# Moving the large on-chip buffers of a three-stage kernel to 128-byte boundaries

## What is computed

```python
# attention: a = softmax(q k^T / 8 + bias) over global and local keys; x = a v
# experts (xc: the tokens whose skip score is positive)
logits = xc @ w_gate; e_idx = argmax(logits); gate_w = softmax(logits)[e_idx]
h = np.maximum(xc[mask] @ w1[e], 0.0)            # 512 -> 1024
y[mask] = gate_w[mask, None] * (h @ w2[e])       # 1024 -> 512
out[do_compute] = xc + y
# gated layer
gate = 1.0 / (1.0 + np.exp(-(x @ w_gate)))       # 512 -> 1536
val = x @ w_val
return (gate * val @ w_out).astype(np.float32)   # 1536 -> 512
```

## The kernel before

| buffers | byte of the line before | after |
|---|---|---|
| `w1h`, `w1l`, `w2h`, `w2l`, all of `gat`, `wraw`, `xq` | 32 | 0 |
| `sTh`, `sTl`, `hTh`, `hTl` | 96 | 0 |
| `srow`, `rrow` (start) | 32, 64 | 0, 32 |
| `at_spot`, `lasth` | 32 | 0 |
| `lastl`, `heads_x`, `bias_win`, `bias_0` | 0 | 96 |
| `raw`, `vs`, `score0` to `score2`, `prob0`, `prob1`, `probT0`, `probT1` | 64 | 32 |
| `score3`, `prob2`, `prob3`, `turner` (start) | 32 | 0 |
| `ident`, `before`, `ones` | 0 | 0 |

## Time and profile before

### The profile page before, as it was taken

The page is one execution under the profiler, slowest core; times in us unless marked ns, Lnnn a source line. Parts: engine busy times, 40 slices in busy tenths (PEclk is TensorE's granted clock), DMA queues, the critical chain, the costliest instruction groups (busy, mean ns, idle before and its releaser), DMA issues.

```text
span 954.6 us, 16759 instructions
## 1 busy us (share of the span) xinstructions
PE 942.3 (99%) x5615; PEld 799.3 (84%) x5616; DVE 648.4 (68%) x1497; ACT 510.8 (54%) x1084; POOL 209.8 (22%) x247
## 2 busy tenths in 40 slices
PE   8999999999999999999999999999999999999998
PEld 6888888989999999788888888888888888888887
DVE  7877787755764465686768774777776846766653
ACT  6988898344443243464545564545454634444442
POOL 2415426422111112113232000222210013232100
PEclk9999999999999999999999999999999999999999
DMA  7787875797876274532121343421213431110342
GB/s 260 263 300 270 326 247 187 274 345 278 282 248 230 94 250 164 177 111 66 47 65 47 91 132 127 157 67 45 67 56 93 133 126 58 53 58 12 88 141 91
DMA packets 59660, 146.14 MB, mean 153 GB/s; under 512 B 6336, under 2 KB 12480, under 8 KB 59584
## 3 DMA queue, kind: packets, MB, share of 16 engines
q1 hardware_dynamic: 52624, 120.92, 37.9%
q0 software_dynamic: 6960, 24.27, 7.4%
HBM read 116.77 MB, written 28.40 MB: 152 GB/s over the span
## 4 chain that ended last, share of the span: by engine, by line
PE 91%; DMA 4%; DVE 2%; issue 1%; ACT 1%; SPq 0%; DVEq 0%; POOLq 0%; ACTq 0%
PE bank L2137 35%; PE bank L1866 14%; PE bank L1868 14%; PE bank L1867 13%; PE bank L1882 4%; PE bank L1909 4%; PE bank L1892 3%; PE bank L1925 2%; DMA vs<-in_own_prev_dram 1%; DMA row_table<-pad 1%; PE bank L2065 1%; PE bank L2127 1%; DMA srow<-row_table 1%; ACT prob L1594 1%; DVE score L940 1%
## 5 line engine op out<-in xcount | busy, mean ns | idle before, releaser
L2137 PE MATMUL bank<-xh,ws_h 128*128 128x512 f32 x490 | 190.6, 389 | 0.0
L2137 PE MATMUL bank<-xl,ws_h 128*128 128x512 f32 x490 | 190.6, 389 | 0.0
L2137 PE MATMUL bank<-xh,ws_l 128*128 128x512 f32 x490 | 190.6, 389 | 0.0
L874 POOL TENSOR_TENSOR p<-p,p 128x512 f32<-128x512 f32 x35 | 46.3, 1323 | 388.3 <-DVE p L1495 388.3
L1866 PE MATMUL bank<-woh,hh 128*128 128x512 f32 x288 | 112.9, 392 | 0.0
L1868 PE MATMUL bank<-woh,hl 128*128 128x512 f32 x288 | 112.1, 389 | 0.0
L1867 PE MATMUL bank<-wol,hh 128*128 128x512 f32 x288 | 112.1, 389 | 0.0
L2137 PEld LDWEIGHTS bank<-xh,ws_l 128*128 128x128 f32 x490 | 92.0, 188 | 19.3
L2137 PEld LDWEIGHTS bank<-xl,ws_h 128*128 128x128 f32 x490 | 92.0, 188 | 19.1
L2137 PEld LDWEIGHTS bank<-xh,ws_h 128*128 128x128 f32 x490 | 92.0, 188 | 18.9
L1594 ACT ACTIVATE prob<-score,lowest 128x256 f32<-128x256 f32 (+1 forms) x192 | 91.2, 481 | 6.1 <-DVE lowest L940 6.1
(11 more groups left out here) (272 smaller groups left out, 2018.4 us busy)
## 6 DMA issues: line engine op xcount, KB each, us to landing
wraw<-in_w_dram SPq DMA_DIRECT2D x64, 512.0 KB, 5.5
graw<-in_w_gated_dram SPq DMA_DIRECT2D x36, 512.0 KB, 3.6
woraw<-in_w_out_dram SPq DMA_DIRECT2D x72, 256.0 KB, 2.6
raw<-in_qk_dram SPq DMA_DIRECT2D x48, 336.0 KB, 6.4
vs<-in_own_prev_dram SPq DMA_DIRECT2D x16, 768.0 KB, 5.3
mixed<-xs SPq DMA_DIRECT2D x12, 512.0 KB, 3.2
xq<-mixed SPq DMA_DIRECT2D x12, 512.0 KB, 6.4
out_dram<-ostage SPq DMA_DIRECT2D x22, 256.0 KB, 2.0
```

Source lines behind the costliest of these rows:

```text
L874: pool.tensor_tensor(p7[:], p7[:], p1[:], ALU.add).then_inc(u3_done, 1)
L2137: ins = pe.matmul(bank, w[:, a + k], x[:, q, k], start=(first and k == 0 and i == 0), stop=(k == 1 and i == 2), skip_group_check=not first)
```

## The change

The change moves buffers and nothing else. `SMALL` goes from 7968 to 7936, which is 62 times 128, and so everything that begins at or after it moves 32 bytes down. To make room, `lexp` (216 bytes) leaves the small buffers and gets a place among the attention's; the small buffers behind it move 224 bytes down. The sum of `srow` and `rrow` is rounded up to a multiple of 128 before `sTh`, which puts `sTh`, `sTl`, `hTh` and `hTl` 32 bytes higher than before.

```diff
         UNIT = 8 * KC * FF
-        SMALL = 7968
+        LINE = 128
+        SMALL = 7936
+        assert (BASE + SMALL) % LINE == 0
         SHARED = SMALL + 4 * UNIT
...
         ldiff = small("ldiff", [P, NQ, NE], f32)
-        lexp = small("lexp", [P, NQ, NE + 1], f32)
         lsum = small("lsum", [P, NQ], f32)
...
         place_l = att2("place_l", [P, NQ, 2 * NE + 1], f32)
+        lexp = att2("lexp", [P, NQ, NE + 1], f32)
         so_far = att2("so_far", [P, NQ, NE], f32r)
...
         rrow = moe("rrow", [P, 2, ROW], f32)
+        moe = place(SHARED + 4 * 4 * FF + (4 * 4 * ROW + LINE - 1) // LINE * LINE)
         sTh = moe("sTh", [P, KC, SLOT], f32r)
```

## The result

The changed kernel has a median of 958.1 us (955.9 to 960.3, 20 executions) against 956.6 us (955.3 to 958.1, 20 executions) of the kernel before, measured beside it: ratio 1.0015, 95% interval 1.0008 to 1.0021. It is slightly slower, not faster. The two profiled executions have the same span, 954.6 us, so this difference of 0.15% can't be read from their ends. What the profiles do show is a change in the stretch of the expert phase.

A forecast was written before the change was run, and what follows sets the result against it. From 181 us the matmul engine was taken as the bound: number of matmuls times pitch. Only the second product's -2.56 us counted, all other terms nothing, giving 953.2 us from the median of 955.76 us; range 943 to 958.

The forecast's parts named there:

- the second product's: Experts' 512-column matmuls on `w2h`: pitch to fall 6.67 ns to 226.67 ns, on 384 matmuls 2.56 us saved.
- the first product: Experts' 864 matmuls of 256 columns: relation goes from 64 bytes apart to 0, taken as no change in time.
- the stated end of +2.6 us: First product's slow end: 3 ns more per matmul, if one case of line 2050 carried all its surplus.
- the weight load stands in the way: First product: why 5.8 us less was doubted; a 128-column weight load needs about as long as 256 moving columns.
- The gated layer: Line 2137 and `unit`, 2382 matmuls: both operands move from byte 32 to 0, relation stays, no change; 1 ns is 2.4 us.
- Attention: Its buffers change places in the line; taken as no change, with 1.4 us as the end to either side.
- Nothing changes: Rival: the second product's extra 6.67 ns comes from something other than place in the line; 955.8 us, chance 0.20.
- The start in the line counts by itself: Rival: byte 0 speeds up gated layer and second product by 11.7 us to 944.1 us, far end 916 us; chance 0.20.
- byte 0 is the worse place: Rival: gated layer's weight loads up to 5 ns longer, its pitch 6.67 ns longer, 15.9 us, 971.6 us; chance 0.15.

The follow-up runs named there:

- m1_places: Separate kernel on zeros, not the reference: blocks of 45 matmuls, both operands at byte 0, 32, 64 or 96; same place 226.67 ns at 512 columns, 120.0 ns at 256.
- e3_plus128: Changed kernel with `sTh`, `sTl`, `hTh`, `hTl` 128 bytes higher, distance 0 modulo 256 in both products; ratio 0.9995 to the kernel before.
- experiment 1: The same run as m1_places; its diagonal is the four pairs with both operands at the same place, 226.67 ns at 512 columns.
- Experiment 5: Kernel of m1_places with one stationary operand and the moving one 0 to 1024 bytes further; 226.7 to 234.3 ns at 512 columns, 113.3 to 120.0 ns at 256.

## Why the prediction was wrong

**The step that failed** is the second product's: "After the change `hTh` and `w2h` both stand at byte 0: the same relation as in line 2137 today." They do stand at byte 0 of a 128-byte line, but 128 bytes apart modulo 256, while line 2137 has 0. That the relation of the two operands counts and not their place was right; the period was taken from the change's own constant instead of from a row, and so the step gave the second product a relation that it doesn't get. Of the expected 6.67 ns, 0.8 came. The relation isn't symmetric either: +64 and -64 differ by 4.4 ns at 512 columns (m1_places). With the relation that the step meant (e3_plus128) the pitch is 226.67 ns in steady state as forecast, and the 512-column distances fall by 2.5 us.

**The second error** is a term of the sum: the first product, "at 256 columns the relation hardly counts. I take nothing." The pitch ranges from 113.3 to 120.0 ns over the distances, nearly as wide as at 512 columns. The change cost 1.6 us here, inside the stated end of +2.6 us. The row it was judged by, line 2050, happened to lie near the kernel's own 117.7 ns: its distances are 0 and 160 modulo 256 and not "0 and 32", they are the same after the change, and it has 118.3 ns in some profiles and 120.0 in others. The argument against a gain, "the weight load stands in the way", was too strong: 113.3 ns was reached in other layouts, 4.4 ns below the 117.7 of before.

**The other parts.** The gated layer: unchanged to the last digit, as said (its distance is 0 modulo 256 on both sides). Attention: within the profile's spread, as said. *Nothing changes* came out nearest in time, but not by its reason, since two pitches moved in opposite directions. *The start in the line counts by itself* and *byte 0 is the worse place* fell with line 2140's 114.24 us at another place and with the diagonal of experiment 1. For the last, the 192 ns of the weight loads of `ones` were no matter of byte 0: those of `hTh` at byte 0 take 187 to 193 ns, a median of 188. The measured 958.1 us lies just above the range of 943 to 958. Part of that is the base: the kernel before had 956.6 us beside it, 0.9 above the 955.76 that the forecast started from. The rest is the sign: +1.5 us where -2.56 was forecast.

By the Trainium skill (TensorE: Matmul & The Clock Gate, "Step-by-step: what each phase is for") the weight load and the running matmul read through ports of their own, and loading takes nothing from the matmul's reads. Experiment 5 speaks against it: with no other engine at work and only the distance of the two operands changed, the pitch moved by up to 7.6 ns at 512 columns and 6.7 ns at 256, at a granted clock of 1.00. Where in the chip the two meet, no run shows.

## What to carry to other kernels

Where weight loads alternate with matmuls back to back, look at the distance of moving and stationary operand modulo 256 bytes before aligning anything: 0 was best for 512 columns and, with 96, worst for 256. An alignment to a round number is no goal in itself; 128 bytes left it to chance which half of the 256 the partner fell on. Judge a layout by the pitch from start to start in the profile of each product, not by one that was measured alone, since the state of a product can depend on what runs before it; and then look for the wait that a shorter product uncovers.

## What was not expected of the hardware

- The pitch of float32r matmuls depends on the operands' distance with a period of 256 bytes: 226.7 to 234.3 ns for 512 columns, 113.3 to 120.0 ns for 256, and no distance is best for both.
- The sign counts: +64 has 228.9 ns and -64 has 233.3 ns at 512 columns.
- Two steady states at the same distance: 113.3 and 117.8 ns at 192 with 256 columns, 117.3 and 118.7 at 160; 118.7 and 120.0 ns at 128 in different slots of one kernel; 118.3 and 120.0 ns for line 2053 in two executions of one program.
- What in the chip makes the period, and what sets the state, stays open. Distances below 32 bytes, other widths, other types and other gaps between blocks were not tried. Nor was a layout found that has 113.3 and 226.7 ns together in all slots.
